# A retention, feed-forward and routed-expert kernel: the expert tiles turned by VectorE's 32x32 blocks and small on-chip transfers, not by TensorE

## The reference, cut to what matters

```python
def reference(q, k, v, moe_w_in, moe_w_out, w_gate, w_noise, noise, w1, w2):
    # q, k, v: 4 x 8 heads x 576 x 64
    ret = (q @ k.T / 8) * Dmat                 # Dmat: gamma_h ** (i - j) for i >= j, else 0
    x = heads_side_by_side(ret @ v)            # 2304 tokens x 512
    h = x @ moe_w_in                           # 512 x 2048
    x = softplus(h) @ moe_w_out                # 2048 x 512
    noisy = x @ w_gate + log1p(exp(x @ w_noise)) * noise      # 2304 x 8
    two largest experts of each token, softmax over the two as weights
    for e in range(8):                         # w1[e]: 512 x 1024, w2[e]: 1024 x 512
        out[tokens of e] += weight * (relu(x[tokens of e] @ w1[e]) @ w2[e])
```

## Time and profile before

| | |
|---|---|
| median of the runs | 1004.03 us |
| the profiled execution | 1005.6 us |
| its span | 1003.8 us |
| TensorE matmuls | 990.3 us busy (99%) |
| ScalarE | 425.3 us (42%) |
| VectorE | 404.2 us (40%) |
| GpSimd | 205.2 us (20%) |
| DMA | 97.67 MB, 97 GB/s in the mean |

### The profile page before, as it was taken

The page is one execution under the profiler, slowest core; times in us unless marked ns, Lnnn a source line. Parts: engine busy times, 40 slices in busy tenths (PEclk is TensorE's granted clock), DMA queues, the critical chain, the costliest instruction groups (busy, mean ns, idle before and its releaser), DMA issues.

```text
span 1003.8 us, 21683 instructions
## 1 busy us (share of the span) xinstructions
PE 990.3 (99%) x5856; PEld 854.0 (85%) x5857; DVE 404.2 (40%) x803; ACT 425.3 (42%) x727; POOL 205.2 (20%) x198
## 2 busy tenths in 40 slices
PE   9899999999999999999999999999999999999997
PEld 8789998998998998989788888888888888888886
DVE  3665533432433434446563222243366464222222
ACT  2237755554555455567522222232365453222221
POOL 4540000020010200200333222222212232222222
PEclk9999999999999999999999999999999999999999
DMA  9963450000000000053316222243267451212211
GB/s 304 298 198 127 139 205 1 1 32 1 1 32 0 0 31 0 13 209 126 84 38 228 64 71 62 65 154 127 88 239 251 136 178 59 73 55 63 63 43 35
DMA packets 48380, 97.67 MB, mean 97 GB/s; under 512 B 19389, under 2 KB 24893, under 8 KB 44224
## 3 DMA queue, kind: packets, MB, share of 16 engines
q1 hardware_dynamic: 25536, 68.59, 19.8%
q0 software_dynamic: 10992, 27.84, 8.8%
q10 hardware_dynamic: 11808, 0.68, 0.8%
HBM read 81.31 MB, written 20.37 MB: 101 GB/s over the span
## 4 chain that ended last, share of the span: by engine, by line
PE 93%; DVE 2%; issue 2%; ACT 1%; DMA 1%; ACTq 0%; DVEq 0%; POOL 0%; POOLq 0%
PE bank L789 27%; PE bank L791 27%; PE bank L790 27%; PE bank L935 3%; PE bank L881 2%; PE bank L739 2%; PE bank L713 1%; PE bank L732 1%; PE bank L839 1%; PE bank L752 1%; PE bank L694 0%; DVE sco L1321 0%; DMA xg<-x_rows,meta_x 0%; PE bank L846 0%; DMA square<-c_sq 0%
## 5 line engine op out<-in xcount | busy, mean ns | idle before, releaser
L789 PE MATMUL bank<-ew,xgT_hi 128*128 (+1 forms) x328 | 131.5, 401 | 0.0
L789 PE MATMUL bank<-xs_hi,mw 128*128 128x384 f32 x384 | 129.9, 338 | 0.0
L791 PE MATMUL bank<-xs_hi,mw 128*128 128x384 f32 x384 | 129.5, 337 | 0.0
L790 PE MATMUL bank<-xs_lo,mw 128*128 128x384 f32 x384 | 128.9, 336 | 0.0
L789 PE MATMUL bank<-ew,hT_hi 128*128 (+1 forms) x320 | 128.3, 401 | 0.3 <-DVE hT_lo L1604 0.3
L791 PE MATMUL bank<-ew,xgT_lo 128*128 (+1 forms) x328 | 128.2, 391 | 0.0
L790 PE MATMUL bank<-ew,xgT_hi 128*128 (+1 forms) x328 | 127.8, 390 | 0.0
L791 PE MATMUL bank<-ew,hT_lo 128*128 (+1 forms) x320 | 125.1, 391 | 0.0
L790 PE MATMUL bank<-ew,hT_hi 128*128 (+1 forms) x320 | 124.8, 390 | 0.0
L789 PE MATMUL bank<-mw,g_hi 128*128 128x512 f32 x288 | 114.6, 398 | 0.0
L791 PE MATMUL bank<-mw,g_lo 128*128 128x512 f32 x288 | 113.7, 395 | 0.0
(11 more groups left out here) (229 smaller groups left out, 1695.5 us busy)
## 6 DMA issues: line engine op xcount, KB each, us to landing
raw<-w_ex SPq DMA_DIRECT2D x32, 1024.0 KB, 4.8
stage<-w_ff SPq DMA_DIRECT2D x16, 512.0 KB, 3.3
out<-blank SPq DMA_DIRECT2D x3, 1536.0 KB, 11.1
x_rows<-x2sb SPq DMA_DIRECT2D x6, 768.0 KB, 4.2
kbuf<-kN SPq DMA_DIRECT2D x16, 256.0 KB, 4.5
vbuf<-vN SPq DMA_DIRECT2D x16, 256.0 KB, 5.4
qbuf<-qT SPq DMA_DIRECT2D x15, 256.0 KB, 4.9
kTd<-kT SPq DMA_DIRECT2D x9, 256.0 KB, 6.4
```

The lines of the kernel that those rows point to most:

```text
L789: pe.matmul(o, a_hi, b_hi, start=first, stop=False)
L790: pe.matmul(o, a_hi, b_lo, start=False, stop=False)
L791: return pe.matmul(o, a_lo, b_hi, start=False, stop=last)
```

## The change

VectorE turns 32x32 blocks (`dve.transpose`): of the gathered rows in SBUF (`turn_x`) into `turned_x`, and of the first product, straight out of its bank in two halves (`turn_hidden`), into `hid`. After that each block is turned in itself but lies on the partitions of its tokens. Four transfers of 64 KB for a tile of x, and four for each half of a hidden tile, issued by SP (`move_x`, `move_hidden`), carry the blocks to the partitions of their features (`x_there`, `h_there`), as 128 rows of 512 bytes each. ScalarE's and VectorE's splits read from there with a step of four elements (`landed`), and the relu is in these splits: `ACT.Relu` for the high part, a maximum with zero for the low one. ScalarE's `relu` is gone, as are TensorE's turns from tile 4 and hidden 2 on; those of the first tiles stay. In the loops the loads of the weights are issued by ScalarE, behind its weight splits; the first few stay with SP. The buffers of the last hidden tile move to where `raw` was.

```diff
+        h_there, a = place("h_there", [P, 2, 4 * P], F32, a)
+        x_there, a = place("x_there", [P, 4 * P], F32, a)
+        assert a <= R_C
+        turned_x, _ = place("turned_x", [P, D], F32, R_W - D * 4)
+        hE_hi, a = place("hE_hi", [P, FT2, P], F32R, R_X)
+        hE_lo, a = place("hE_lo", [P, FT2, P], F32R, a)
+        assert a <= R_X + 4 * QUARTER * 4
...
+        def landed(ap):
+            return ap.rearrange("p (t c) -> p c t", c=4)
...
+        def load_weights(eng, g, p):
+            for q in range(2):
+                with eng.If(entry2(eng, T_LOAD[q], g, 0, 1)):
+                    e = entry(eng, T_E, g, 0, E - 3)
+                    expert = entry2(eng, T_NEXT, g, 0, E - 1)
+                    eng.wait_ge(w_lo_done[p], e * 2 + q + 3)
+                    load_raw(eng, expert, p, q)
...
+            def move_x(g):
+                sp.wait_ge(xgT_made, g + 1)
+                for i in range(4):
+                    sp.dma_start(x_there[:, i * P:(i + 1) * P], turned_x[32 * i:32 * i + 32, :].rearrange("a (j n) -> a j n", j=4)
+                                 ).then_inc(x_moved, 16)
+            def move_hidden(g, h):
+                sp.wait_ge(h_turned, g * 2 + h + 1)
+                for i in range(4):
+                    sp.dma_start(h_there[:, h, i * P:(i + 1) * P],
+                                 hid[32 * i:32 * i + 32, h * 512:(h + 1) * 512].rearrange("a (j n) -> a j n", j=4)
+                                 ).then_inc(h_moved[h], 16)
             sp.wait_ge(tab2_done, 1)
             alone(sp, got_x[1], 32)
-            load_weights(0, 0)
+            load_weights(sp, 0, 0)
+            load_weights(sp, 1, 0)
+            sp.wait_ge(x2_stored, 16 * NCH)
+            for h in range(2):
+                sp.sem_inc(h_moved[h], 64)
+            sp.sem_inc(x_moved, 192)
+            move_hidden(2, 0)
+            move_hidden(2, 1)
+            load_weights(sp, 0, 1)
+            load_weights(sp, 2, 0)
+            load_weights(sp, 1, 1)
             pair = entry(sp, T_PAIR, 0, PAIR_LOW, PAIR_HIGH)
-            with sp.Fori(0, pair) as i:
+            with sp.Fori(1, pair) as i:
                 for s in range(2):
-                    load_weights(2 * i + s + 1, 0)
-                    load_weights(2 * i + s, 1)
+                    g = 2 * i + s
+                    move_x(g + 2)
+                    move_hidden(g + 1, 0)
+                    move_hidden(g + 1, 1)
+            with sp.If(entry(sp, T_TWO, 0, 0, 1)):
+                move_hidden(2 * pair + 1, 0)
+                move_hidden(2 * pair + 1, 1)
...
-                at_least(pe, relu_done, g)
-                expert_in_part(s, par, 0, range(KT))
+                pe.wait_ge(h_turned, g * 2)
+                expert_in_part(s, par, 0, range(KT)).then_inc(in_half, 1)
                 expert_in_part(s, par, 1, range(KT)).then_inc(m1_done, 1)
...
             def step(i, s, this, after):
                 g = 2 * i + s
-                hidden_transpose(g)
                 expert_in(g + 1, 1 - s, *after)
-                tile_transpose(g + 2, s, i + 2)
                 expert_out(g, *this)
...
-            def relu(g):
-                act.wait_ge(m1_done, g + 1)
-                at_least(act, hT_made, g)
-                nc.scalar.activation(hid[:, 0:512], m1_ps[0], ACT.Relu)
-                nc.scalar.activation(hid[:, 512:1024], m1_ps[1], ACT.Relu).then_inc(relu_done, 1)
-            def split_hidden(g, done=0, h_hi=hT_hi):
+            def split_hidden(g):
                 act.wait_ge(hT_made, g + 1)
+                at_least(act, m2_done, g)
+                for k in range(2):
+                    nc.scalar.activation(hT_hi[:, 4 * k:4 * k + 4, :], hT_ps[k], ACT.Copy).then_inc(hT_hi_done, 1)
+            def split_moved(g, done, h_hi=hT_hi):
                 if done is not None:
-                    at_least(act, m2_done, done)
-                for k in range(2):
-                    nc.scalar.activation(h_hi[:, 4 * k:4 * k + 4, :], hT_ps[k], ACT.Copy).then_inc(hT_hi_done, 1)
+                    act.wait_ge(m2_done, done)
+                for h in range(2):
+                    act.wait_ge(h_moved[h], g * 64)
+                    nc.scalar.activation(h_hi[:, 4 * h:4 * h + 4, :], landed(h_there[:, h, :]), ACT.Relu
+                                         ).then_inc(hT_hi_done, 1)
+            def split_moved_x(g, s, done):
+                act.wait_ge(x_moved, g * 64)
+                act.wait_ge(m1_done, done)
+                nc.scalar.activation(xgT_hi[:, s, :, :], landed(x_there[:, :]), ACT.Copy
+                                     ).then_inc(xgT_hi_done, 1)
...
-            def next_tile(i, s):
-                g = 2 * i + s
-                relu(g + 1)
-                split_weights(g, 1)
+            def next_rows(i, s):
                 alone(act, sent_y[1 - s], (i + s) * 16)
-                load_meta(act, meta_y, 1 - s, g + 1, ld_my[1 - s])
+                load_meta(act, meta_y, 1 - s, 2 * i + s + 1, ld_my[1 - s])
             def step(i, s):
                 g = 2 * i + s
                 alone(act, got_x[s], i * 16 + 32)
                 load_meta(act, meta_x, s, g + 4, ld_mx[s])
-                split_hidden(g, g)
+                split_moved(g, g)
                 split_weights(g + 1, 0)
-                split_tile(g + 2, s)
-                next_tile(i, s)
+                split_moved_x(g + 2, s, g + 1)
+                split_weights(g, 1)
+                load_weights(act, g + 1, 0)
+                load_weights(act, g, 1)
+                next_rows(i, s)
             def split_second(p, q):
...
-            split_hidden(2 * pair, None, hE_hi)
+            for p in range(2):
+                act.wait_ge(w_lo_done[p], 2 * E)
+            split_moved(2 * pair, None, hE_hi)
             with act.If(entry(act, T_TWO, 0, 0, 1)):
-                split_weights(2 * pair + 1, 0)
-                next_tile(pair, 0)
-                split_hidden(2 * pair + 1, 2 * pair)
+                next_rows(pair, 0)
+                split_moved(2 * pair + 1, 2 * pair)
...
+            def turn_x(g, s, count):
+                dve.wait_ge(got_x[s], count * 16)
+                dve.transpose(turned_x[:, :].rearrange("p (j b c) -> p j c b", j=4, b=32),
+                              xg[:, s, :].rearrange("p (c a j) -> p j c a", j=4, a=32)).then_inc(xgT_made, 1)
+            def turn_hidden(g, h):
+                if h == 0:
+                    dve.wait_ge(in_half, g + 1)
+                else:
+                    dve.wait_ge(m1_done, g + 1)
+                dve.transpose(hid[:, h * 512:(h + 1) * 512].rearrange("p (j b c) -> p j c b", j=4, b=32),
+                              m1_ps[h].rearrange("p (c a j) -> p j c a", j=4, a=32)).then_inc(h_turned, 1)
+            def split_moved_x(g, s):
+                dve.wait_ge(xgT_hi_done, g + 1)
+                dve.tensor_tensor(xgT_lo[:, s, :, :], landed(x_there[:, :]), as32(xgT_hi[:, s, :, :]), ALU.subtract).then_inc(xgT_lo_done, 1)
+            def split_moved(g, h_hi=hT_hi, h_lo=hT_lo):
+                for h in range(2):
+                    dve.wait_ge(hT_hi_done, 2 * g + h + 1)
+                    k = slice(4 * h, 4 * h + 4)
+                    dve.scalar_tensor_tensor(h_lo[:, k, :], landed(h_there[:, h, :]), 0.0, as32(h_hi[:, k, :]),
+                                             ALU.max, ALU.subtract
+                                             ).then_inc(hT_lo_done, 1)
...
+            dve.sem_inc(h_turned, 4)
+            turn_hidden(2, 0)
+            turn_hidden(2, 1)
...
             def step(i, s, end=False):
                 g = 2 * i + s
-                split_hidden(g)
+                split_moved(g)
+                turn_x(g + 2, s, i + 2)
+                turn_hidden(g + 1, 0)
                 split_weights(g + 1, 0)
-                split_tile(g + 2, s)
+                turn_hidden(g + 1, 1)
+                split_moved_x(g + 2, s)
                 split_weights(g, 1)
                 if end:
-                    split_hidden(g + 1, hE_hi, [t[:, :, :] for t in hE_lo])
+                    split_moved(g + 1, hE_hi, hE_lo)
                 add_output(i, s)
```

More of the change, by code:

```diff
@@ L320, in build @@
         m1_done, relu_done, hT_made = sem("m1_done"), sem("relu_done"), sem("hT_made")
+        h_turned, x_moved = sem("h_turned"), sem("x_moved")
+        h_moved = [sem(f"h_moved{h}") for h in range(2)]
         hT_hi_done, hT_lo_done, m2_done, y_done = (sem(n) for n in ("hT_hi_done", "hT_lo_done", "m2_done", "y_done"))
@@ L489, in _ @@
                 for q in range(2):
-                    load_raw(first, p, q)
+                    load_raw(sp, first, p, q)
             sp.wait_ge(rec_sent, 16 * 2 * TJ * LEAD_CHUNKS)
@@ L501, in _ @@
                     sp.wait_ge(w_lo_done[p], q + 1)
-                    load_raw(second, p, q)
+                    load_raw(sp, second, p, q)
                 if p == 0:
@@ L513, in _ @@
```

(45 more changed lines are left out.)

35 lines of the change are left out of this document (14 added, 21 removed).

## The result

The changed kernel takes 1313.57 us (median of 4 runs, 1312.81 to 1314.26), the kernel before 1003.98 us on the same chip: a ratio of 1.3081, 95% interval 1.3058 to 1.3103. The profiled execution had a span of 1310.8 us. The forecast was 1132 us and a range of 1070 to 1200: the side was right, the size was not. 180 us are missing from the sum.

The account below looks back on a forecast made before the run. TensorE was taken to bound the kernel before, and a new ring of waits through ScalarE, VectorE and SP after. Head 555 + 37 x 13.5 + weights 64 + tail 13 = 1131.5 us, so about 1132, range 1070 to 1200.

Parts of the forecast that it names:

- the new ring: Loop of waits from ScalarE's hidden split through VectorE, SP's moves and ScalarE's queue: 13.5 us a step, bounds 12.4 to 16.2.
- The head: Start of the expert stage: SP's later move of tile 4 puts ScalarE's next hidden split at 555 us, from 538.03.
- the four conditions: Conditions asked by ScalarE's two load_weights calls in each step: 3.2 us, bounds 2.9 to 3.2.
- the landing: Time for SP's tile transfers to arrive on chip: 2.1 us, bounds 1.7 to 3.7.
- half to half: From ScalarE's half of the hidden split to VectorE's half: 0.63 us.
- VectorE's pair: VectorE's two halves of the hidden split: 1.29 us, of which the next instruction overlaps 0.08.
- the turn: VectorE's turn of the tile (turn_x): 0.70 us, bounds 0.6 to 1.4.
- The weights' 64 us: Time added by weights on ScalarE: second-layer splits 25 us, loads 34, waits 5; together 64, bounds 55 and 75.
- The tail: From the last hidden split to the end of the span: 13.1 us, against 14.45 before the change.
- Faster: Rival: the ring closes in under 11.0 us and TensorE stays the bound, 970 us in all; chance 0.08.
- Slow transfers: Rival: the moves land in 5 us or more, ring above 16, 1261 us in all; chance 0.10.
- The clock falls: Rival: TensorE idles and falls to 1.2 GHz, a step takes 22 us, 1382 us in all; chance 0.04.

Follow-up runs that it names:

- e10: Changed kernel with the tile turn first, weight loads on SP, runs of 32 elements, and the hidden matrix in four 128 KB transfers: 1049.63 us.
- e2: Changed kernel with the weight loads issued by SP behind its moves instead of by ScalarE: 1101.76 us, ratio 1.0981.
- e6: e2 with 160 semaphore increments under a never-true condition added at the end of ScalarE's loop: 1204.29 us, ratio 1.2003.
- e3: Changed kernel with turns writing and splits reading runs of 32 elements instead of one element in four: 1281.36 us, ratio 1.2756.
- e1: Changed kernel with VectorE turning the tile ahead of its halves of the hidden split: 1178.02 us, ratio 1.1716.
- e11: e10 with the first half of each weight load issued by ScalarE again, the second still by SP: 1155.73 us, ratio 1.153.

## Why the prediction was wrong

**Right.** TensorE bound the kernel, a step without the turns would take 11.0 us (e10: 11.0 to 11.1), and the new ring decides instead: every link is in the chain of the changed kernel. The ring's cover is gone in the way described, ScalarE's tile split waits for the transfer and the hidden split for "issue". The head was met within 1 us (554.29 for 555), in part by luck: the first tile's split came 1.2 us earlier than taken (546.77 for 548) and the rest of ScalarE's queue took 7.52 us for 7.2. Moved to SP, the four conditions gave back 3.2 us of an even step (e2), as priced, and the landing is 2.14 us (from 653.63 on in the chain), where 2.1 was taken. A single read took 0.28 us, under the floor of about 600 ns that the prediction gives from the Trainium skill, "DMA: Bandwidth & Descriptors" (section "Latency and other measured facts"); the condition as a whole keeps its 0.8.

**The step that failed is the ring's length**, the sum of 13.5 us, in two ways.

- *A term that isn't in it, 80 us or somewhat more.* `load_weights` twice was priced by what it executes. Its other price is its length: the loop outgrew what ScalarE holds, and each jump back waits for code. No row of the trace of before shows that, since there the loop fitted; but the rule quoted above was to be had, and no rival was made of it. e6 isolates it: 102.5 us for a condition and the code behind it that never runs. The bounds of the ring, 12.4 to 16.2, took in the short step and missed the mean of 18.1 over short and long steps.
- *Terms too small, 90 us.* By the timelines above, in the order of the sum: half to half 1.14 for 0.63; VectorE's pair 2.00 for 1.21; the turn 1.12 for 0.70; SP's wake 0.03 for 0.18; four issues 651.75 to 653.63, 1.88 for 1.44; landing and dispatch 2.25 for 2.10; tile split to next hidden split 7.51 for 7.25. The differences are 0.51, 0.79, 0.42, -0.15, 0.44, 0.15 and 0.26, together 2.42. The first two are one mistake: the pair's duration came from reads of a bank without a step, and the change reads SBUF with a step of four elements. The diff shows that in `landed`; e3 takes the step away, and ScalarE's split is back at 0.63 us and the tile's low part at 0.69. The bound "strided at half rate" was put on the turn alone. There it held: the turn took 1.12 us, inside 0.6 to 1.4, and it too reads with a step of four; the central 0.70, from small turns and a rate without a step, was too low.

The weights' 64 us (71 measured) were nearly right. The tail came out 15.9 us for 13.1. By the timeline 1.0 of it is the strided halves (the first matmul stands at 1297.22, 2.34 us behind the hidden split, for 1.3) and 1.8 is the clock: the last 24 matmuls took 7.3 us for 5.5, the first eight of them mostly 0.43 us apart.

**The rivals.** *Faster*: no step without weights but the last, which has no jump back (14.6 us), was under 15.8 us. *Slow transfers*: the time was nearer to it (1261) than to the sum, but by another cause; the landing is 2.09 to 2.47 us in every step. *The clock falls*: it fell, 0.901 over the run, and with a price in e1, but in the changed kernel the ring hides it up to the tail: TensorE is busy 79% of the span and waits 206.5 us for the hidden's low half. The case as stated, 22 us in each step, didn't come. Of the signs that were named, the tile split's wait ends in the transfer and the hidden split's in "issue", as foretold; the hidden splits stood 15.9 and 20.4 us apart, not 13.5, and TensorE's share was 79%, not about 85%.

## What to carry to other kernels

Taking 1.3 us a step from the engine that is the bound is worth that only where the work put in its place closes no ring; follow each new wait around until it comes back, and price every link with a row of the same kind of access. Count the instructions that a change adds to a loop, also those under a condition that is never true: past some length each jump back is a fetch, here 4.5 to 5 us. And a ring that holds at 11.0 us without other work need not hold beside it: the variant with the lowest time lost its gain in the steps with weights, where the turn stands behind VectorE's weight parts, the moves behind SP's loads, and the moves land later. How much each weighs stayed open.

## What the runs showed of the hardware

- ScalarE's loop of 206 (e2) to 209 (before) listed instructions was repeated without a fetch (18 and 19 instruction packets over the run); with some 273 (e11), with 340 (changed kernel), and with 206 and 160 skipped ones (e6) each pass fetched anew (108 to 110 packets, 4.5 to 5 us a pass).
- A 128x512 fp32 read in SBUF with a step of four elements took 1.1 us on ScalarE and 1.06 on VectorE; in runs of 32 elements, 0.63 and 0.69.
- VectorE's 32x32 turn of 128x512 fp32, read with a step of four elements, took 1.07 to 1.21 us out of SBUF, however it was written, and out of a bank 0.64 with runs of 32 written, 0.98 with a step of four (pairs of 1.27 and 1.96 us).
- Four transfers of 64 KB on the chip were issued 0.62 us apart and landed 2.09 to 2.47 us after the last was issued (changed kernel, 37 steps); in the chain of e10 from 650 to 911 us, among the weight loads, it was 3.12 to 4.70 us in seven of eight cases. With 128 KB each they were issued at the same pace (2.50 us for four, e10).
- After a gap of 6.15 us TensorE's matmuls started 0.43 us apart at a granted clock of 0.50 (e1); in a stretch without gaps, 560 to 640 us of e10, the granted clock was 1.00.
